# An attention and two-layer kernel: SBUF places of TensorE's streamed operands, counted from their weights

## The reference

```python
def _attn_ref(q, k, v, proj):
    q_bits = np.einsum('bhsd,dk->bhsk', q, proj) > 0
    k_bits = np.einsum('bhsd,dk->bhsk', k, proj) > 0
    ...
    mask = q_bucket[:, :, :, None] == k_bucket[:, :, None, :]
    scores = scale * np.matmul(q, k.transpose(0, 1, 3, 2))
    scores = np.where(mask, scores, -1000000000.0)
    attn = np.exp(scores - np.max(scores, axis=-1, keepdims=True))
    attn = attn / (np.sum(attn, axis=-1, keepdims=True) + 1e-09)
    return np.matmul(attn, v)

def _moe_ref(x, w_val, conv_w, w_out):          # conv of 5 taps over tokens
    ...
    gate = 1.0 / (1.0 + np.exp(-gate_pre))
    return gate * (x @ w_val) @ w_out

def _moe2_ref(x, mu_k, mu_r, w_k, w_v, w_r):    # d_ff = 1024
    xk = mu_k * x + (1.0 - mu_k) * x_prev
    xr = mu_r * x + (1.0 - mu_r) * x_prev
    k = np.maximum(xk @ w_k, 0.0)
    v = k * k @ w_v
    r = 1.0 / (1.0 + np.exp(-(xr @ w_r)))
    return r * v
```

## Time and profile before

| | us |
|---|---|
| median of 3 runs | 484.28 (484.23 to 484.29) |
| profiled execution | 484.03 |
| its span, first to last instruction | 482.2 |
| busy: PE / PEld | 472.4 / 401.4 |
| busy: DVE / ACT / POOL | 345.7 / 279.4 / 259.8 |

### The profile page before, as it was taken

The page is one execution under the profiler, slowest core; times in us unless marked ns, Lnnn a source line. Parts: engine busy times, 40 slices in busy tenths (PEclk is TensorE's granted clock), DMA queues, the critical chain, the costliest instruction groups (busy, mean ns, idle before and its releaser), DMA issues.

```text
span 482.2 us, 9492 instructions
## 1 busy us (share of the span) xinstructions
PE 472.4 (98%) x3541; PEld 401.4 (83%) x3541; DVE 345.7 (72%) x607; ACT 279.4 (58%) x597; POOL 259.8 (54%) x258
## 2 busy tenths in 40 slices
PE   7899999999999999999999999999999999999997
PEld 6766767676676776777779999999999999999997
DVE  5887897988888888887747977876678579326211
ACT  5977878878787987876745541442443353344230
POOL 5795647374472745652197673575455457346140
PEclk9999999999999999999999999999999999999999
DMA  6210310304021030200220001001000000100101
GB/s 231 67 55 18 113 41 5 135 17 137 16 68 72 17 136 18 71 19 18 88 87 1 3 1 44 1 1 46 2 2 32 13 2 1 45 1 2 44 1 44
DMA packets 10557, 20.69 MB, mean 43 GB/s; under 512 B 1680, under 2 KB 6928, under 8 KB 10512
## 3 DMA queue, kind: packets, MB, share of 16 engines
q1 hardware_dynamic: 10224, 19.94, 12.4%
q10 hardware_dynamic: 288, 0.15, 0.1%
HBM read 16.94 MB, written 3.15 MB: 42 GB/s over the span
## 4 chain that ended last, share of the span: by engine, by line
PE 79%; DVE 9%; issue 5%; ACT 3%; POOL 2%; DMA 1%; SPq 0%; DVEq 0%; POOLq 0%; ACTq 0%
PE ps L735 29%; PE ps L723 14%; PE ps L743 12%; PE ps L699 10%; PE ps L688 10%; ACT probs L500 2%; PE ps L709 2%; DVE gate L923 1%; DVE tmp_b L1014 1%; DVE negmax L880 1%; DVE pt L887 1%; PE ps L671 1%; DVE x L913 1%; PE ps L662 1%; DMA raw_k<-kT 1%
## 5 line engine op out<-in xcount | busy, mean ns | idle before, releaser
L880 DVE TENSOR_REDUCE negmax<-ps 128x1 f32<-128x768 f32 x96 | 91.7, 956 | 23.6 <-PE ps L688 22.9
L688 PE MATMUL ps<-k,q 128*128 128x384 f32 x384 | 92.1, 361 | 3.4 <-ACT probs L500 2.8
L500 ACT ACTIVATE probs<-ps,negmax 128x768 f32<-128x768 f32 x96 | 86.6, 902 | 10.2 <-DVE negmax L880 9.9
L699 PE MATMUL ps<-ident,probs 128*128 128x128 f32 x576 | 82.3, 275 | 1.2
L699 PEld LDWEIGHTS ps<-ident,probs 128*128 128x128 f32 x576 | 66.8, 140 | 11.9 <-DVE pt L887 4.7
L688 PEld LDWEIGHTS ps<-k,q 128*128 128x128 f32 x384 | 62.7, 189 | 15.3 <-ACT probs L500 10.6
L723 PE MATMUL ps<-pt,vals 128*64 128x384 f32 x384 | 68.8, 494 | 0.0
L450 POOL TENSOR_TENSOR h_lo<-tmp_b,h_hi 128x256 fp32r<-128x256 f32 x48 | 38.9, 816 | 45.3 <-ACT h_hi L602 45.3
L508 ACT ACTIVATE pt<-ps 128x384 f32<-128x384 f32 x96 | 47.0, 489 | 18.7 <-PE ps L699 15.0
L887 DVE COPY pt<-ps 128x384 f32<-128x384 f32 x96 | 52.1, 542 | 2.8 <-PE ps L699 2.8
L735 PE MATMUL ps<-xk_hi,w_hi 128*128 128x256 f32 x192 | 53.7, 280 | 0.0
(11 more groups left out here) (86 smaller groups left out, 1105.4 us busy)
## 6 DMA issues: line engine op xcount, KB each, us to landing
w_raw<-w SPq DMA_DIRECT2D x8, 640.0 KB, 6.4
raw_q<-qT SPq DMA_DIRECT2D x8, 384.0 KB, 5.2
raw_k<-kT SPq DMA_DIRECT2D x8, 384.0 KB, 3.2
vals<-v SPq DMA_DIRECT2D x16, 192.0 KB, 2.4
out<-w_raw SPq DMA_DIRECT2D x24, 128.0 KB, 1.7
w_raw<-w SPq DMA_DIRECT2D x4, 512.0 KB, 3.3
codes_b<-codes ACTq DMA_DIRECT2D x1, 128.0 KB, 4.2
proj_bd<-proj ACTq DMA_DIRECT2D x1, 16.0 KB, 3.3
```

Source lines behind the costliest of these rows:

```text
L500: act.activation(probs[par][:, :], score[par], ACT.Exp, bias=negmax[:, t:t + 1], accum_out=sums[:, t, 0:1]).then_inc(exp_done, 1)
L688: last = pe.matmul(ps[:, 2 * par + half, 0:HALF], qq[h][:, q], kk[h][:, half * HALF:(half + 1) * HALF], start=first, stop=not first)
L699: last = pe.transpose(tbank[u][:, k * P:(k + 1) * P], probs[g % 2][:, kt * P:(kt + 1) * P], ident[:, :])
L880: dve.tensor_reduce(negmax[:, t:t + 1], score[g % 2], AX.XY, ALU.max, negate=True).then_inc(max_done, 1)
```

## The change

Unused tensors get other sizes, the order of the tensors of a set becomes q1, q2, (unused), k1, k2, and 64 unused bytes after the three sets bring their total to a multiple of 512. Nothing but addresses changes.

```diff
+KEYS_BEHIND = (96, 160, 192)
...
-        def apart(name, size):
+        def apart(name, size, stack=ctx):
-            sb(f"apart_{name}", [P, size // 4])
+            sb(f"apart_{name}", [P, size // 4], F32, stack)
...
         for n in range(SETS):
             s = (NHEADS + n) % SETS
             q1[s] = sb(f"q1_{s}", [P, SEQ], F32R, att)
+            q2[s] = sb(f"q2_{s}", [P, SEQ], F32R, att)
+            apart(f"k_{s}", KEYS_BEHIND[s], att)
             k1[s] = sb(f"k1_{s}", [P, SEQ], F32R, att)
-            q2[s] = sb(f"q2_{s}", [P, SEQ], F32R, att)
             k2[s] = sb(f"k2_{s}", [P, SEQ], F32R, att)
+        apart("sets", -sum(KEYS_BEHIND) % 512, att)
...
-        apart("x", 256)
+        apart("x", 320)
...
-        apart("y", 448)
+        apart("y", 32)
...
-        apart("h", 288)
+        apart("h", 160)
...
-        apart("xk", 32)
+        apart("xk", 416)
...
-        apart("xr", 288)
+        apart("xr", 64)
```

## The result

The changed kernel takes 485.46 us (median; 485.27 to 486.11) against 484.28 for the kernel before: ratio 1.0022, 95% interval 1.0013 to 1.0031. It is slower by about a quarter of a per cent. Its profiled execution took 485.27 us, with a span of 483.5.

What follows compares the result with a forecast made beforehand. The prediction took TensorE's start-to-start matmul spacing, set by operand-to-weight distance, to bound the kernel. Its stage terms summed to -1.3 us from 484.28, giving 482.9 us on the median's scale, with a range of 477.6 to 487.6.

Steps and rivals of the forecast that it cites:

- the period of 128 bytes: Dense stages and keys: spacing repeats every 128 bytes of distance (streamed start minus weight start), giving every new place a relative.
- the size of the spacing at place 0: Dense stages: place 0, scaled from the attention scores by columns, was taken as 116.7 ns a matmul.
- xk at 192 as 64: xk stage, 576 matmuls: new distance 192 behaves like 64, 116.7 to 113.4 ns, -1.90 us.
- h at 160 as 32: h stage, 576 matmuls: new distance 160 behaves like 32, stays at 116.7 ns, 0 us.
- y at 128 and xr at 256 as 0: y and xr stages go to 116.7 ns: y -0.43 us; xr +0.79 in five chunks, -0.06 in the first.
- x at 96 as 480: x stage, 288 matmuls: new distance 96 behaves like 480, 116.9 to 118.2 ns, +0.37 us.
- keys: Attention scores: set 0 slower by +0.30 us, set 1 unchanged, set 2 faster by -0.41, together -0.1 us.
- All of it is on the path: All stages: the whole sum of -1.3 us moves the end, as nothing but TensorE is late there.
- B: Rival, dense stages and keys: period 256, only places 224 to 32 collide; -6.8 us, median 477.5; chance 0.18.
- C: Rival, xk, h and xr stages: new places fall into the slow 118 ns pattern; +3.3 us, median 487.5; chance 0.23.
- point of decision: xk and h stages: a mean above 117.0 ns makes the kernel slower by over 0.97 us.
- D: Rival, all stages: spacing belongs to stage order and beginnings, not place; time stays at 484.3 us; chance 0.22.

Runs made afterwards that it cites:

- xk_only: Kernel before with only the xk stage's distance between streamed operand and weights moved, to 192: 484.5 us, ratio 1.0006.
- all_192: Kernel before with all five dense stages (x, y, h, xk, xr) at distance 192, keys as before: 484.03 us, ratio 0.9988.
- places_rest: Kernel before with untried distances: x 320, y 352, h 384, xk 448, xr 416, keys 32, 64, 128: 486.43 us, ratio 1.0038.
- all_0: Kernel before with all five dense stages at distance 0: 490.18 us (one execution).
- keys_only: Kernel before with only the keys' part of the change (distances 96, 160, 192), dense stages as before: 484.62 us, ratio 0.9999.
- w1_moved: Kernel before with weights w1 moved by 32 bytes, streamed tensors and w2 left where they were: 486.51 us (one execution).
- w2_level: x32_rest192 with weights w2 at the same place modulo 512 as w1, every streamed tensor but x at 192: 481.58 us, ratio 0.9949.
- x32_rest192: Kernel before with x at distance 32 and the other four dense stages at 192, keys as before: 482.49 us, ratio 0.9956.

## Why the prediction went wrong

It forecast 482.9 us and faster; the time is 485.46, inside its range of 477.6 to 487.6, on the other side of before. The reading of the bound was right: the spacing of TensorE's matmuls moved the end, and the addresses of the other engines' operands cost nothing that the waits show. So was the view to take it from. Two steps failed: the period of 128 bytes, and the size of the spacing at place 0. Term by term:

- xk at 192 as 64: 113.4 forecast, 113.4 measured, -1.9 us. Right: 64 and 192 are the pair for which a period of 128 works. That it held in all six chunks was in part luck: at 192 the same stage had 117.8 ns in two chunks of xk_only and in five of all_192. Whether x at 96 ahead of it is what kept it fast, no run shows.
- h at 160 as 32: 116.7 forecast, 118.7 measured in five of six chunks. This is the largest miss of one stage, +1.1 us. The failed step is the period: the rows allowed 256 as well as 128, and 128 was taken because it gave every place a relative. places_rest shows that 256 holds and 128 does not; 160 had no relative among the rows of before.
- y at 128 and xr at 256 as 0, and 0 as 116.7: measured 118.8 and 119.6, together +1.4 us against the forecast. The failed step is the sizing of place 0. It was scaled from the scores by their columns, and all_0 has 120.0 for it. For xr the relative was right, as 256 behaves as 0, and only the value was wrong; for y the period was wrong too, as 128 isn't 0.
- x at 96 as 480: 118.2 forecast, 119.9 measured, +0.5 us. The direction was right.
- keys: -0.1 forecast, nothing measured (keys_only). The sum was right by the cancelling of terms that weren't there: no set moved as forecast. The dense stages' classes don't carry over to the scores.
- the path: "All of it is on the path" failed for the stages up to the wait for `recept` at 317 us. Of the +1.8 us of the stages 0.6 went into shorter pauses.

From -1.3: 1.1 + 1.4 + 0.5 + 0.1 is +3.1 and gives +1.8; less the 0.6 of pauses it is +1.2, against 1.3 in the span.

One reading was off and changed no term: at 109 ns for 128 columns the transposes run at a little over half the rate of the dense stages (1.17 against 2.19 columns a ns), and not at less than half.

The rivals: B (distance from 0 is what counts) was right on the period and on 192, which can be as good as 64, and wrong on the rest, as 96, 128 and 160 are among the slowest. C had the sign. Its point of decision was wrong: h and xk have a mean of 116.0, under its 117.0, and the kernel is slower all the same, since x, y and xr came to +2.5 where the forecast had +0.67. D is refuted by w1_moved and all_0; but its observation, that place 64 showed two spacings, was half of the matter. The prediction saw that, and took it for a risk of one stage rather than for a state that passes from stage to stage.

By the Trainium skill's rule of two independent read ports ("TensorE: Matmul & The Clock Gate", "Step-by-step: what each phase is for"), as the prediction reads it, all kernels that differ in addresses alone would be equal. all_0 and w2_level differ in nothing else and are 8.6 us apart, so the measurement decides against it as a rule for the time; whether it is at these ports that the two streams meet, no run shows. The Trainium skill's formula for a matmul by itself (same page, "Back-to-back issue gap") gives 109.2 ns; the best sustained here, with a load beside each matmul, is 113.3.

## What to carry to other kernels

Where TensorE's back-to-back stream is the bound, measure the distance between starts, stage by stage, and the distance of streamed operand and weights in memory: between the worst and the best place lay 6% of a matmul here (120.0 and 113.3 ns). Don't interpolate between places, and don't judge a place by one stage: look at every occurrence, since a place can have a fast and a slow pattern, and what comes before the stage has a part in which it is. Another place for one stage (here x at 32) ahead of a run of stages at one good distance did better than the same good place everywhere (x32_rest192 against all_192, with intervals that don't overlap). And look for the next wait: what a faster TensorE gains ahead of it is lost there.

## What the runs showed of the hardware

For float32r matmuls of 256 columns with 128x128 weights, at the full granted clock, the spacing by distance modulo 256 bytes was: 0, 119.6 to 120.0 ns; 32, 116.7 or 117.8; 64, 113.4 or 117.8; 96, 119.9; 128, 118.8 or 120.1; 160, 118.7 or 117.4; 192, 113.4 or 117.8; 224 (tried as 480 only), 118.3. A pattern goes on across hundreds of matmuls and across stages at one distance; after a pause (starts 0.2 to 1.3 us apart), one short matmul or a seam of another distance it can be the other one. Loads of a half and a quarter of the columns leave the spacing between 113 and 120 ns. At distances 16 bytes off these steps it was 116.7 to 119.3 ns, in one execution. What couples the two streams is open.
